# The second batch's values summed over four rows by accumulating DMAs on Pool's queue instead of by Pool's additions

## What is computed

```python
B, H, S, D = q.shape          # 2, 8, 576, 64
factor = 4
Sd = S // factor              # 144
q_d = q.reshape(B, H, Sd, factor, D).mean(axis=3)
k_d = k.reshape(B, H, Sd, factor, D).mean(axis=3)
v_d = v.reshape(B, H, Sd, factor, D).mean(axis=3)
out_d = sm_attn(q_d, k_d, v_d)
...
return (out_up + out_local)   # out_up: out_d repeated 4 times; out_local: a band of 7 keys
x = moe(x)                    # silu(x @ w_gate) * (x @ w_val) @ w_out
return moe2(x)                # Sinkhorn-weighted sum over 8 experts
```

## Time and profile before

| | us |
|---|---|
| median of 3 runs | 1106.4 (1105.56 to 1106.45) |
| profiled execution, its own time | 1104.89 |
| its span, first to last instruction | 1103.1 |
| PE busy in the span | 1088.6 |
| DVE busy | 644.3 |
| ACT busy | 375.8 |
| POOL busy | 34.4 |

### The profile page before, as it was taken

How to read it: one execution, slowest core, us unless ns; L and a number is a source line. 1 busy time by engine, 2 the same in 40 slices (tenths; PEclk the granted TensorE clock), 3 DMA queues, 4 the chain that set the end, 5 groups by cost and what they waited for, 6 DMA issues and landing times.

```text
span 1103.1 us, 17767 instructions
## 1 busy us (share of the span) xinstructions
PE 1088.6 (99%) x6970; PEld 999.8 (91%) x6970; DVE 644.3 (58%) x1112; ACT 375.8 (34%) x607; POOL 34.4 (3%) x36
## 2 busy tenths in 40 slices
PE   8989999999999999999999999999999999999998
PEld 5879999999998988998998899899889889989987
DVE  5676665556558875664475375557437636644742
ACT  2336664344324431332242142223223313322321
POOL 3440000000000000000000000000000000000000
PEclk7569999999999999999999999999999999999999
DMA  7353112222230210120030021012002101200111
GB/s 185 111 181 87 64 43 68 77 77 67 72 109 21 77 39 20 58 77 20 19 106 27 0 85 48 19 53 80 19 19 76 39 18 57 76 19 19 38 38 48
DMA packets 30225, 64.98 MB, mean 59 GB/s; under 512 B 12396, under 2 KB 14700, under 8 KB 30188
## 3 DMA queue, kind: packets, MB, share of 16 engines
q1 hardware_dynamic: 30188, 64.47, 18.8%
HBM read 62.10 MB, written 2.36 MB: 58 GB/s over the span
## 4 chain that ended last, share of the span: by engine, by line
PE 95%; DVE 3%; DMA 1%; issue 1%; ACT 1%; SPq 0%; DVEq 0%
PE ps L1140 56%; PE ps L1420 31%; PE ps L1212 2%; PE ps L1167 2%; PE ps L1181 1%; PE ps L1217 1%; DMA kt<-kT 1%; PE ps L1229 1%; PE ps L1161 1%; PE ps L1192 0%; DVE w_lo L707 0%; DVE x_lo L707 0%; DVE xf L904 0%; SPq L343 0%; DVE h L1074 0%
## 5 line engine op out<-in xcount | busy, mean ns | idle before, releaser
L1140 PE MATMUL ps<-w_hi,h_hi 128*128 128x512 f32 x576 | 224.4, 390 | 0.0
L1140 PE MATMUL ps<-w_lo,h_hi 128*128 128x512 f32 x576 | 224.2, 389 | 0.0
L1140 PE MATMUL ps<-w_hi,h_lo 128*128 128x512 f32 x576 | 224.2, 389 | 0.0
L642 ACT ACTIVATE h_hi<-h 128x1024 fp32r<-128x1024 f32 (+1 forms) x80 | 77.2, 975 | 253.7 <-PE ps L1140 218.2
L1020 DVE SCALAR_TENSOR_TENSOR acc<-ps,prob_e,acc 128x512 f32<-128x512 f32 x63 | 47.3, 750 | 190.6 <-PE ps L1140 190.6
L1420 PE MATMUL ps<-x_hi,w_hi 128*128 128x288 f32 x512 | 151.2, 295 | 1.0 <-DVE x_lo L707 1.0
L1420 PE MATMUL ps<-x_hi,w_lo 128*128 128x288 f32 x512 | 150.8, 294 | 0.0
L1420 PE MATMUL ps<-x_lo,w_hi 128*128 128x288 f32 x512 | 150.6, 294 | 0.0
L1140 PEld LDWEIGHTS ps<-w_hi,h_lo 128*128 128x128 f32 x576 | 108.1, 188 | 22.4
L1140 PEld LDWEIGHTS ps<-w_lo,h_hi 128*128 128x128 f32 x576 | 108.1, 188 | 22.2
L1140 PEld LDWEIGHTS ps<-w_hi,h_hi 128*128 128x128 f32 x576 | 108.1, 188 | 22.0
(11 more groups left out here) (133 smaller groups left out, 1757.7 us busy)
## 6 DMA issues: line engine op xcount, KB each, us to landing
raw<-w SPq DMA_DIRECT2D x64, 512.0 KB, 3.5
raw<-w_up SPq DMA_DIRECT2D x24, 512.0 KB, 3.6
raw<-w_out SPq DMA_DIRECT2D x16, 384.0 KB, 2.9
vw<-v SPq DMA_DIRECT2D x10, 252.0 KB
qt<-qT SPq DMA_DIRECT2D x4, 576.0 KB, 5.3
kt<-kT SPq DMA_DIRECT2D x4, 576.0 KB, 6.4
v<-v SPq DMA_DIRECT2D x8, 288.0 KB
out<-acc SPq DMA_DIRECT2D x9, 256.0 KB, 2.0
```

Source lines behind the costliest of these rows:

```text
L642: nc.scalar.activation(h2_hi[:, idx % 2, f0:f1, :], h2[:, f0:f1, t * P:(t + 1) * P], ACT.Relu).then_inc(h2_hi_ready, 1)
L1140: done = nc.tensor.matmul(dst, a, b, start=first and n == 0, stop=last and n == len(terms) - 1)
```

## The change

Nothing is changed for the first batch. For the second, SP no longer loads the raw copy `v4` (four DMAs of 288 KB). POOL's four additions for chunks 2 and 3 go too. In their place POOL issues 16 DMAs after the four `ring_lo` subtractions and ahead of the `sum_queries`. For each head group there are four rounds, one for each of the four rows that are summed. A round is two DMAs from `v` in HBM straight into `vd`. The first round writes, and the other three add to what is there. Each adding round waits until the two DMAs of the round before have landed. A DMA moves 72 partitions by 4 heads by 64 numbers, 72 KB in 288 pieces of 256 bytes.

```diff
+        v_gather = [sem(f"v_gather{hh}") for hh in range(2)]
...
-            for c in range(2, B * 2):
-                sp.wait_ge(v_sum, 2 * c)
-                load_v4(c)
             load_queries(1, 0)
...
+            def gather_values(c):
+                b, hh = divmod(c, 2)
+                heads = slice(hh * DM // 2, (hh + 1) * DM // 2)
+                for r in range(POOL):
+                    if r:
+                        pool.wait_ge(v_gather[hh], 16 * QC * r)
+                    for kc in range(QC):
+                        rows = slice(kc * S // QC, (kc + 1) * S // QC)
+                        src = v[b, rows, heads].rearrange("(p r) (h d) -> p r h d", r=POOL, d=D)[:, r]
+                        dst = vd[:, kc, hh * HALF:(hh + 1) * HALF, 0:D]
+                        if r:
+                            nc.gpsimd.dma_start(dst, src, accum_op=ALU.add).then_inc(v_gather[hh], 16)
+                        else:
+                            nc.gpsimd.dma_start(dst, src).then_inc(v_gather[hh], 16)
...
-            for c in range(B * 2):
+            for c in range(2):
                 sum_values(c)
             for n in range(SLOTS):
                 pool.wait_ge(w_hi, n + 1)
                 ...
+            pool.wait_ge(o_ready, DOWNS)
+            for c in range(2, 2 * B):
+                gather_values(c)
             for n in range(4):
                 sum_queries(n // 2, n, *((qt, qd, q_load) if n % 2 == 0 else (kt, kd, k_load)))
...
-                if kind == "down":
-                    pe.wait_ge(v_sum, 2 * (2 * b + hh + 1))
+                if kind == "down" and b:
+                    pe.wait_ge(v_gather[hh], 16 * QC * POOL)
+                elif kind == "down":
+                    pe.wait_ge(v_sum, 2 * (hh + 1))
```

## The result

The changed kernel takes 1128.8 us (median of 4 runs, 1126.3 to 1130.0) against 1106.4 (4 runs, 1105.6 to 1108.1). The ratio is 1.020, with a 95% interval of 1.018 to 1.022: slower by 2.0%. The forecast was 1127 us in a range of 1112 to 1143. The profiled execution took 1126.3 us with a span of 1124.1, 21.0 us longer than the span before.

A forecast was written before the change was run, and what follows sets the result against it. PE, busy 99% of the span, bounds the kernel. Unit 14's scores 19.3 us late plus 1.4 low clock give 20.7 on the profiled 1104.9, so 1125.6; the median's 1.5 more makes 1127 us, range 1112 to 1143.

The forecast's parts named there:

- The slack and its user: POOL ends its second `sum_queries` at 75.19 us, PE needs it for unit 14's scores at 82.93: 7.7 us spare.
- The start: POOL's DMAs begin after the last `ring_lo`, at 59.2 us, where POOL was free at 62.1 before.
- The issues: POOL issues 16 DMAs at 1.2 us each, between SP's 0.79 and 1.51: 19.2 us.
- The landings: POOL waits for six landings at 3.3 us each, low end 2.0, high end 6.4: 19.8 us.
- The sum of the three: On POOL, 59.2 + 19.2 + 19.8: the DMA block ends at 98.2 us.
- The sums of queries and keys: POOL's first two `sum_queries` add 4.0 us after the DMAs; unit 14's scores start at 102.2 instead of 82.93.
- The low clock: After PE's gap at unit 14 the clock is low for 3 us of MLP work, costing 1.4 us.
- The side gain: First batch: without the additions, `ring_lo` no longer run in a row holding DVE; 1.9 to 5.0 us, hidden in PE's wait.
- The cheap rounds: POOL issues like SP, landings take 2 to 2.5 us, PE 4 to 9 us late: 1112.7 to 1116 us; chance 0.17.
- the low sum: POOL's block at 16 × 0.79 + 6 × 2.0 = 24.6 us, unit 14's scores 4.9 late: 1112.7 us.
- the estimate of 17.4 us for eight rounds: From the Trainium skill's figures, a round on POOL costs 2.2 us all in, and PE would not wait at all.
- rival 3: Issues run beside landings, a round costs 2.0 us, PE does not wait or waits briefly: 1104.5 or 1102.8 us; chance 0.05.

The follow-up runs named there:

- halved DMAs: The changed kernel with every DMA cut in two, 32 of 144 pieces instead of 16 of 288: 1137.8 us (ratio 1.030).
- plain ones: The changed kernel with every round writing instead of adding, so the sum is left out: 1122.0 us (ratio 1.015).
- SP's loads held: The changed kernel with SP holding back weight chunks 4 to 7 and the second batch's windows until head group 1's third round landed: 1120.6 us (ratio 1.012).
- kernel without the DMAs: The changed kernel without the 16 DMAs and PE's waits on them, leaving out the second batch's downsampled values: 1099.2 us (ratio 0.994).
- moved `ring_lo`: The kernel before with POOL's first `ring_lo` ahead of its sums for chunk 3; run twice: 1099.9 and 1101.2 us (ratio 0.996 both times).
- paced DMAs: The changed kernel with head group 0's DMAs before all `ring_lo`, group 1's after `sum_queries`, each `ring_lo` awaiting one more `x_lo`: 1096.3 us (ratio 0.990).
- additions behind `sum_queries`: The kernel before with POOL's additions for chunks 2 and 3 behind `sum_queries`, each `ring_lo` awaiting one more `x_lo`: 1099.0 us (ratio 0.995).

## Why the prediction was right

**The slack and its user** were right: the 7.7 us before unit 14's scores were used up, the only new wait of PE is the one for POOL's `kd`, and behind it nothing recovers.

**The start** was put at 59.2 us and was 55.95, since the clock rose early and the casts came sooner. **The issues** were put at 1.2 us each, 19.2 in all, and held POOL for 16.5. The row that I took as the upper end, 1.51 us for 1008 pieces on SP, was no guide: the halved DMAs show that POOL's issue does not go by the pieces, and the plain ones that 0.7 us of it is the DMA and the rest the adding. **The landings** were put at 3.3 us each, 19.8 in all, and took 24.4, in two kinds: 2.05 to 2.37 in free queues, and 11.1 and 4.5 in full ones. I had spread one middle value over both. The worst one is 1.7 times the 6.4 us that I took as the high end. **The sum of the three** came out at 96.9 us against 98.2: errors of 3.3, 2.7 and 4.6 us, the last of the other sign. That 1127 lies so near 1128.8 is in part this luck. The start varies with the clock, too: in three versions with the same first batch (plain rounds, SP's loads held, halved DMAs) the DMAs began at 57.3, 58.8 and 58.0 us, and the profiled execution here is the shortest of the four runs.

**The sums of queries and keys** took 4.9 us instead of 4.0, the first one begun while the last issue still ran, and unit 14's scores came at 101.9 where I had 102.2. **The low clock** was put at 1.4 us for 3 us and cost 2.0, scores of unit 14 included; it lasted until 106.5, 4.6 us.

**The side gain** has the right mechanism, and its size only in part. I had 1.9 to 5.0 us, hidden in the wait. Hidden it was: the kernel without the DMAs brought 6 to 7 us to light, and the moved `ring_lo` 4 to 6. In the changed kernel's profile PE reached unit 14 10.7 us earlier. The 5.0 rests on a misread row: until 53 us the clock was low before the change, so the step of 3.43 us from 50.97 to 54.40 is no step at the high level. At the high level the scores of units 9 to 13 start 2.4 to 3.0 us apart (46.00, 48.41, 51.17, 54.18 and 57.07 in the changed kernel). And the held DVE cost the clock that had just risen. From the kernel before, PE and the clock by stretch, and PE's wait behind the held `x_lo`:

```profile
53.00:54.00 1.00, 1.00 (x11) 0.89 0.00 0
55.00:56.00 1.00, 0.09 (x2) 1.00 0.00 0
57.00:58.00 1.00, 0.00 (x0) 0.50 0.00 0
```
```profile
58.53 1.06 PE L1181 MATMUL ps<-ident,e_t 120*126 120x120 f32 x4 [3.44 <-ACT e_t L470]
```

Without that gap the clock stays high through the rest of the first batch and shortens every step. How much this gives goes with the time of the rise: PE was at unit 14 10.7 us earlier with the rise at 45 us, 7.2 at 53 (the first one with the moved `ring_lo`), and 5.3 at 55 (without the DMAs).

**The rivals.** The cheap rounds fell: even in free queues a round costs 4.77 and 4.74 us from issue to issue (85.95, 90.72, 95.46), where the low sum has 2 × 0.79 + 2.0 = 3.6. The landings there were as cheap as that rival had them; the adding issues were not, and neither were the landings in full queues, as said against it. The Trainium skill ("DMA: Bandwidth & Descriptors", Anatomy of one DMA — SWDGE (gpsimd) path) has about 2.0 us fixed for a DMA from this engine. The trace agrees for the landing alone, 2.05 to 2.37 us. Counted all in, as in the estimate of 17.4 us for eight rounds, it leaves out that POOL is held for another 2.4 us by a pair that adds. That estimate also took the bytes of one DMA for a round of two; with both, the same figures make an estimate of 18.7 us for eight rounds, past the 17.5 that rival 3 allowed.

**Open.** The paced DMAs gave 1096.3 us, the additions behind `sum_queries` 1099.0. The intervals of their ratios do not overlap (0.989 to 0.992 and 0.993 to 0.998), but they were measured on two chips, with 5 and 12 runs. The traces place the difference. From the start of unit 14's scores to the end, the span is 1020.1 to 1020.3 us in the kernel before and in the profiles of every version in which PE waits neither for POOL nor for a DMA there, with DMAs, with additions and without either: behind that point neither way of summing costs anything. The two profiles differ by 1.4 us, and so do the starts of these scores (75.55 and 76.95). The first batch reads the same in both (longest `x_lo` 1.08 and 0.73 us) but for the clock, which rose at 49 and at 54 us. The single times follow the mean granted clock: of the twelve runs with the additions, the fastest took 1093.8 us at 0.987 and the slowest 1107.6 at 0.972. When the clock rises in the first batch is not set by the kernel alone, and I have no experiment that sets it. So it isn't shown that the DMAs are better than well-placed additions, only that well placed they cost PE nothing behind unit 14's scores.

## What to carry to other kernels

An accumulating DMA from POOL is not free of POOL: a chain of n rounds holds the queue for n issues and the n - 1 landings between them, here 4.75 us a round with nothing else in the queues. Put such a chain where its engine has nothing behind it that others wait for, and price each landing by what the DMA engines carry at that time.

When a change takes work off an engine, look at what closes up behind it and at what it used to hold. Here most of what the freed POOL was worth could be had by moving one instruction: 4 to 6 us of the 6 to 7. And when several versions differ by a few us, look for a point from which all their traces take the same time: it says where the difference can't be.

## What the runs showed of the hardware that I had not expected

- A DMA issued by POOL holds it 0.7 to 0.8 us if it only writes (1.41 to 1.66 for a pair), and 1.2 us if it adds (2.37 to 2.43 for a pair), for 288 pieces; with 144 pieces each, four that add take 4.55 us and four that write 2.98, so about the same per DMA.
- A DVE subtraction with two SBUF inputs that meets a row of POOL subtractions waits for the whole row, not for one: 4.79 us in a row of three, 10.14 us in a row of four and the sum behind it, 0.40 alone. The Trainium skill ("SBUF — State Buffer", Who interferes with whom) has the exclusion, for one instruction against another. The traces add that POOL, with the next one ready, keeps its turn. Where the next POOL instruction had to wait 0.07 or 0.08 us for the one before it, DVE came through: the 1.64 us of the moved `ring_lo` end between two additions. In the eight cases in these traces of an `x_lo` held in the first batch for over 1.5 us, it ends 0.25 to 0.28 us after the POOL instruction that held it.
- TensorE's granted clock in the first batch rose at 53 us in the kernel before, fell at about 57 after the held DVE, and rose for good near 74. In the changed kernel it rose at 45 and stayed until PE's long wait; in one version it was high from about 11 us to 48.5. The same kernel differs by up to 14 us from run to run with it.
- A landing of 147 KB took 11.1 us while SP issued 5.7 MB of loads around it, and 5.3 with 2.3 MB of queries and keys alone.
